# Turning x and the keys of a fused attention and gated kernel on VectorE and through a DRAM scratch instead of on TensorE

## The reference

```python
# r, k, v: (4, 8, 768, 48); w in 0.8..0.95; u: (8, 48)
for t in range(S):
    cur = einsum('bhd,bhe->bhde', u[None] * kt, vt)
    y[:, :, t] = einsum('bhd,bhde->bhe', rt, state + cur)
    state = wt[:, :, :, None] * state + einsum('bhd,bhe->bhde', kt, vt)
x = y.transpose(0, 2, 1, 3).reshape(3072, 384)
xn = x / sqrt(mean(x * x) + 1e-6) * rms_g
x = (silu(xn @ w_gate) * (xn @ w_val)) @ w_out      # 384 -> 1536 -> 384
out = (s * max(x @ w_in, 0) ** 2 + b) @ w_out2      # 384 -> 2048 -> 384
```

## Time and profile before

| | |
|---|---|
| median of 3 runs | 1022.48 us (1021.54 to 1025.43) |
| profiled execution | 1021.45 us |
| its span, first to last instruction | 1019.3 us |
| PE busy | 996.5 us, 98% |
| DVE busy | 523.2 us, 51% |
| ACT busy | 331.4 us, 33% |
| POOL busy | 266.2 us, 26% |
| DMA | 66.12 MB, mean 65 GB/s |
| granted TensorE clock | 1.00 |

### The profile page before, as it was taken

The page is one execution under the profiler, slowest core; times in us unless marked ns, Lnnn a source line. Parts: engine busy times, 40 slices in busy tenths (PEclk is TensorE's granted clock), DMA queues, the critical chain, the costliest instruction groups (busy, mean ns, idle before and its releaser), DMA issues.

```text
span 1019.3 us, 24567 instructions
## 1 busy us (share of the span) xinstructions
PE 996.5 (98%) x10614; PEld 863.9 (85%) x10614; DVE 523.2 (51%) x702; ACT 331.4 (33%) x565; POOL 266.2 (26%) x189
## 2 busy tenths in 40 slices
PE   5899999999999999999999999999999999999998
PEld 5778888888888888888888888898998989989898
DVE  6889836763776477547742225506327054161340
ACT  1442332233223312231323445505226043151340
POOL 4555723551454156316710550000000000000000
PEclk9999999999999999999999999999999999999999
DMA  7570240114013301420104311001010010100000
GB/s 265 163 285 10 83 161 32 49 46 158 33 48 96 138 5 48 147 88 3 49 3 176 103 32 63 0 24 39 17 46 0 23 39 8 54 0 15 15 8 23
DMA packets 21978, 66.12 MB, mean 65 GB/s; under 512 B 2944, under 2 KB 6272, under 8 KB 20608
## 3 DMA queue, kind: packets, MB, share of 16 engines
q1 hardware_dynamic: 21312, 63.65, 17.8%
q10 hardware_dynamic: 576, 1.13, 0.3%
HBM read 55.34 MB, written 9.44 MB: 64 GB/s over the span
## 4 chain that ended last, share of the span: by engine, by line
PE 87%; DVE 1%; issue 0%; ACT 0%; DVEq 0%
PE o_ps L1319 15%; PE o_ps L570 14%; PE value_ps L558 13%; PE gate_ps L558 13%; PE level_ps L47 10%; PE mix_ps L1319 5%; PE gate_ps L47 5%; PE value_ps L47 5%; PE level_ps L430 4%; PE level_ps L504 2%; PE mix_ps L504 2%; PE level_ps L482 1%; PE level_ps L548 0%; PE level_ps L446 0%; PE level_ps L466 0%; PE mix_ps L466 0%
## 5 line engine op out<-in xcount | busy, mean ns | idle before, releaser
L1393 DVE SCALAR_TENSOR_TENSOR sqr<-relu,sb_col 128x512 f32<-128x512 f32 x96 | 72.3, 753 | 216.9 <-ACT relu L1351 216.9
L1108 POOL TENSOR_TENSOR R<-R,arena 128x512 f32<-128x512 f32 x72 | 115.6, 1622 | 196.6 <-PE level_ps L430 175.8
L979 DVE TENSOR_TENSOR u_raw<-value_ps,u_raw 128x512 f32<-128x512 f32 x66 | 45.5, 690 | 126.2 <-PE value_ps L558 126.2
L751 ACT ACTIVATE u_raw<-gate_ps 128x512 f32<-128x512 f32 x72 | 43.0, 598 | 183.4 <-PE gate_ps L558 183.4
L1319 PE MATMUL o_ps<-wt_hi,g_lo 128*128 128x384 f32 x288 | 96.2, 334 | 0.0
L1319 PE MATMUL o_ps<-wt_hi,g_hi 128*128 128x384 f32 x288 | 96.2, 334 | 0.0
L1319 PE MATMUL o_ps<-wt_lo,g_hi 128*128 128x384 f32 x288 | 96.2, 334 | 0.0
L758 ACT ACTIVATE u_hi<-u_raw 128x512 fp32r<-128x512 f32 x66 | 41.7, 632 | 145.6 <-DVE u_raw L979 145.6
L570 PE MATMUL o_ps<-u_hi,wo_hi 128*128 128x512 f32 x216 | 88.4, 409 | 0.0
L558 PE MATMUL value_ps<-x_hi,w_hi 128*128 128x512 f32 x216 | 85.5, 396 | 0.0
L558 PE MATMUL gate_ps<-x_hi,w_hi 128*128 128x512 f32 x216 | 84.7, 392 | 0.7 <-DVE x_lo L952 0.7
(11 more groups left out here) (166 smaller groups left out, 2132.0 us busy)
## 6 DMA issues: line engine op xcount, KB each, us to landing
kr_nat<-kr SPq DMA_DIRECT2D x10, 1152.0 KB, 6.5
K<-kT SPq DMA_DIRECT2D x12, 512.0 KB, 3.9
arena<-wT SPq DMA_DIRECT2D x12, 512.0 KB, 6.7
R<-rT SPq DMA_DIRECT2D x10, 512.0 KB, 4.0
w_raw<-wgv SPq DMA_DIRECT2D x12, 384.0 KB, 6.2
v_sb<-v SPq DMA_DIRECT2D x12, 384.0 KB, 5.2
x_scratch<-x_sb SPq DMA_DIRECT2D x18, 256.0 KB, 2.3
x_raw<-x_scratch SPq DMA_DIRECT2D x6, 768.0 KB, 4.3
```

What stands on the lines that cost most here:

```text
L751: act.activation(u[:, f % 2], gate_ps[:], ACT.Silu).then_inc(silu_done, 1)
L979: dve.tensor_tensor(u[:, f % 2], value_ps[:], u[:, f % 2], ALU.mult).then_inc(u_done, 1)
L1108: pool.tensor_tensor(q, q, decay(blk, l, 0), ALU.mult).then_inc(rmul_done, 1)
L1393: dve.scalar_tensor_tensor(out=sq[f % 2][:], in0=relu[f % 2][:], scalar=sb_col[:, 0:1], in1=relu[f % 2][:], op0=ALU.mult, op1=ALU.mult).th ...
```

## The change

In the stages 1 to 5 neither keys nor x are turned on PE. `turn_keys(s, blk)` on DVE turns 128x1024 keys in blocks of 32 by 32 behind the last key multiplication of each pair (group 18); SP stores the result to `k_scratch` and loads it back in four DMAs of 32 partitions each, which swaps the blocks, 1 KB a piece. KTr is laid out with the pair of heads innermost, so that an update's stationary operand takes every eighth element (`turned_keys`). x goes the same way: `turn(s, blk)`, two DVE operations of 128x384, three stores to `y_scratch` and four loads a pair, in pieces of 256 bytes. The tokens of x then lie in another order (quadrants, blocks inside), which the store of the gated layer's output undoes; the gain g is multiplied in by `upper_x` and `lower_x`. Updates go from behind group 22 to 23, the rest of them and the readings from 24 and 26 to 25 and 27, and what hangs on them. Stage 0 keeps its transposes on PE. Some late weights are split one group earlier.

```diff
-LATE_WEIGHTS = (5, 7, 9, 11, 14, 17, 20, 23, 28)
-LATE_OUT = (8, 13, 16, 21, 27)
+UPDATE_AT, ATTEND_AT, UPPER_AT, NEXT_AT = 23, 25, 33, 34
+LATE_WEIGHTS = (5, 7, 9, 11, 14, 17, 20, 22, 28)
+LATE_OUT = (8, 13, 16, 21, 26)
...
-    KTr = [arena[:, n // C, n % C * NP * P:(n % C + 1) * NP * P] for n in range(CH)]
+    KTr = [arena[:, blk, 0:Q * P] for blk in range(2)]
...
+    def turned_keys(n):
+
+        return KTr[n // C].rearrange("p (d q) -> p d q", q=Q)[:, :, n % C * NP:(n % C + 1) * NP]
+
+    def turned_quadrants(blk):
+
+        return x_raw[:].rearrange("p k (q b f) -> p k q b f", q=QUAD, b=2)[:, :, :, blk]
...
+        def store_turned_keys(s, blk):
+            wait(sp, k_turned, 2 * (s - 1) + blk + 1)
+            wait(sp, kt_in[blk], QUAD * (s - 1) * 16)
+            sp.dma_start(k_dram[blk], KTr[blk].rearrange("p (b f) -> p b f", b=QUAD)).then_inc(kt_stored[blk], 16)
+
+        def load_turned_keys(s, blk):
+            wait(sp, kt_stored[blk], s * 16)
+            for b in range(QUAD):
+                sp.dma_start(KTr[blk][32 * b:32 * b + 32].rearrange("p (a f) -> p a f", a=QUAD),
+                             k_dram[blk, :, b].rearrange("(a i) f -> i a f", a=QUAD)).then_inc(kt_in[blk], 16)
+
+        def store_turned(s, blk):
+            wait(sp, y_turned, CH * (s - 1) + C * blk + C)
+            wait(sp, x_in[blk], QUAD * (s - 1) * 16)
+            for k in range(KT):
+                sp.dma_start(y_dram[blk, k], turned_quadrants(blk)[:, k]).then_inc(y_stored[blk], 16)
+
+        def load_turned(s, blk):
+            wait(sp, y_stored[blk], KT * s * 16)
+            for q in range(QUAD):
+                sp.dma_start(turned_quadrants(blk)[32 * q:32 * q + 32].rearrange("p k q f -> p (k q) f"),
+                             y_dram[blk, :, :, q].rearrange("k (a i) f -> i (k a) f", a=QUAD)).then_inc(x_in[blk], 16)
...
             load_natural(2 * s + 1)
+            for blk in range(2):
+                store_turned_keys(s, blk)
+                load_turned_keys(s, blk)
             if s + 1 < NSB:
                 for blk in range(2):
                     load_keys(s + 1, blk)
...
+            store_turned(s, 0)
+            load_turned(s, 0)
+            store_turned(s, 1)
+            if s + 1 < NSB:
                 load_queries(s + 1, 1)
+            load_turned(s, 1)
+            if s + 1 < NSB:
                 load_values(s + 1, 1)
                 load_natural(2 * s + 2)
...
-            wait(pe, kt_out, turned(CH * s + n) + 1)
-            if n % 2 == 0 and not batch_end(CH * s + n + 1):
-                wait(pe, kt_out, turned(CH * s + n + 1) + (1 if n == 0 else 0))
+            if s == 0:
+                wait(pe, kt_out, 3 if n == 0 else n // 2 * 2 + 2)
+            else:
+                wait(pe, kt_in[blk], QUAD * s * 16)
...
-                                   KTr[n][:, p * P + h * SUB:p * P + (h + 1) * SUB], v_sb[blk][:, c, head * D:(head + 1) * D],
+                                   turned_keys(n)[:, h * SUB:(h + 1) * SUB, p], v_sb[blk][:, c, head * D:(head + 1) * D],
...
         def upper_x(s):
             wait(act, value_done, F1 * s)
+            for blk in range(2):
+                wait(act, x_in[blk], QUAD * s * 16)
             for k in range(KT):
-                wait(act, xe_done, KT * (s - 1) + k + 1)
-                act.activation(x_hi[:, k], x_raw[:, k], ACT.Copy).then_inc(xhi_done, 1)
+                act.activation(x_hi[:, k], x_raw[:, k], ACT.Copy, scale=g_col[:, k:k + 1]).then_inc(xhi_done, 1)
...
+        def turn_keys(s, blk):
+            wait(dve, kmul_done, level_no(s, LV - 1, blk))
+            wait(dve, rmul_done, level_no(s, 1, blk))
+            wait(dve, wb_done, level_no(s, 1, blk))
+            dve.transpose(KTr[blk].rearrange("p (b j q) -> p b q j", b=QUAD, j=32),
+                          K[blk][:].rearrange("p (q b t) -> p b q t", b=QUAD, t=32)).then_inc(k_turned, 1)
+
+        def turn(s, blk):
+            wait(dve, norm_done, CH * s + C * blk + C)
+            wait(dve, xlo_done, split_tiles(s - 1, KT - 1))
+            for c in range(C):
+                out = turned_quadrants(blk).rearrange("p k q (c j) -> p (k q) c j", c=C)[:, :, c]
+                dve.transpose(out, y_sb[C * blk + c][:].rearrange("p (b j) -> p b j", j=32)).then_inc(y_turned, 1)
...
             if k == TOP_AT:
-                keys_after(s, LV - 1)
+                for blk in range(2):
+                    multiply_keys(s, LV - 1, blk)
+                    turn_keys(s, blk)
...
-            if k == 26:
+            if k == ATTEND_AT + 2:
                 normalise(s, 0)
                 attention_out(s, 2)
                 attention_out(s, 3)
-            if k == 28:
+                turn(s, 0)
+            if k == ATTEND_AT + 4:
                 normalise(s, 1)
+                turn(s, 1)
```

More of the change, by code:

```diff
@@ L120, in copied, with by_quadrant, of_block, attention_and_gated_phase @@
     return 2 * (blk + 1) if s == 0 else 2 * (s + 2)
+def by_quadrant(ap, n):
+    return ap.rearrange("p (a n j) -> p a n j", a=QUAD, j=32)[:, :, n]
+def of_block(ap, blk):
+    return ap.rearrange("p (a b f) -> p a b f", a=QUAD, b=2)[:, :, blk]
 def split_tiles(s, k):
     return KT * (s + 1) + k + 1
-def attention_and_gated_phase(nc, block, a, whole, first, x1_dram, x1_out, x_hi, x_lo, const_in_squared, level_ps, mix_ps, gate_ps,
+def attention_and_gated_phase(nc, block, a, whole, first, x1_dram, y_dram, k_dram, x1_out, x_hi, x_lo, const_in_squared, level_ps, mix_ps, gate_ps,
                               value_ps, o01_ps, o_ps):
@@ L221, in attended_ps, with turned_ps @@
         return (first_y_ps if s == 0 else y_ps)[n]
[L223 to L224 removed]
+    def turned_ps(k, blk):
+        return o_ps[k] if blk == 0 else tail_ps[k]
     def natural(b):
@@ L315, in load_keys @@
         def load_keys(s, blk):
-            wait(sp, kt_done, turned(CH * (s - 1) + C * blk + C) if s > 0 else 0)
+            if s == 1:
+                sp.wait_ge(kt_done, C * blk + C)
+            else:
+                wait(sp, k_turned, 2 * (s - 2) + blk + 1)
             sp.dma_start(K[blk][:], a["kT"][2 * s + blk]).then_inc(k_in[blk], 16)
@@ L449, in top_level, with turn_first_keys @@
             mm.then_inc(level_done, 1)
-        def turn_keys(s, n):
-            if batch_end(CH * s + n):
-                return
+        def turn_first_keys(n):
             blk, c = n // C, n % C
[L455 to L458, removed]
+            keys_ready(pe, 0, LV, blk)
+            if n == 3:
                 wait(pe, far_done, copied(0, 0))
[L460 to L463, removed]
             for p in range(NP):
                 q = c * NP + p
-                mm = pe.transpose(keys_ps(s, n)[:, p * P:(p + 1) * P], K[blk][:, q * P:(q + 1) * P], eye[:])
+                mm = pe.transpose(first_kt_ps[n][:, p * P:(p + 1) * P], K[blk][:, q * P:(q + 1) * P], eye[:])
             mm.then_inc(kt_done, 1)
@@ L492, in attend @@
             if blk == 0:
-                wait(pe, kt_out, turned(CH * (s + 1)))
+                wait(pe, kt_out, CH)
+                wait(pe, yo_done, CH * s)
             elif s > 0:
@@ L639, in first_attention @@
             keep_busy(4, gate_ps)
-            turn_x(0, range(0, C))
-            turn_x(0, range(C, CH))
+            first_turn(range(0, C))
+            first_turn(range(C, CH))
             keep_busy(3, gate_ps)
@@ L691, in place_far, with first_keys_out @@
                         act.activation(dst, src[:, :, blk], ACT.Copy).then_inc(far_done, 1)
[L693 to L698, removed]
+        def first_keys_out(n):
+            wait(act, kt_done, n + 1)
+            act.activation(turned_keys(n).rearrange("p d q -> p q d"),
+                           first_kt_ps[n].rearrange("p (q d) -> p q d", q=NP), ACT.Copy).then_inc(kt_out, 1)
         def square(s, n):
@@ L949, in first_lower_x @@
             for k in range(KT):
-                cols = slice(blk * TB, (blk + 1) * TB)
                 wait(dve, xhi_done, KT * blk + k + 1)
-                dve.scalar_tensor_tensor(out=x_lo[:, k, cols], in0=turned_ps(0, k, blk)[:, cols], scalar=g_col[:, k:k + 1],
-                                         in1=x_hi[:, k, cols].bitcast(F32), op0=ALU.mult,
-                                         op1=ALU.subtract).then_inc(xlo_done, 1)
+                dve.scalar_tensor_tensor(out=of_block(x_lo[:, k], blk), in0=of_block(turned_ps(k, blk), blk),
+                                         scalar=g_col[:, k:k + 1], in1=of_block(x_hi[:, k], blk).bitcast(F32),
+                                         op0=ALU.mult, op1=ALU.subtract).then_inc(xlo_done, 1)
         def lower_x(s):
@@ L958, in lower_x, with lower_squared_x @@
                 wait(dve, xhi_done, split_tiles(s, k))
-                dve.tensor_tensor(x_lo[:, k], x_raw[:, k], x_hi[:, k].bitcast(F32), ALU.subtract).then_inc(xlo_done, 1)
+                dve.scalar_tensor_tensor(out=x_lo[:, k], in0=x_raw[:, k], scalar=g_col[:, k:k + 1],
```

(11 more changed lines are left out.)

95 lines of the change are left out of this document (38 added, 57 removed).

## The result

The changed kernel takes 1034.14 us (median of 4 runs, 1033.75 to 1034.53) against 1023.9 (1021.54 to 1025.43, also of 4) for the kernel before on the same chip: ratio 1.0112, 95% interval 1.0096 to 1.0128. It is slower, by 1.1%. The forecast was 1020.5, so its sign is wrong; the stated range, 1010.5 to 1037, holds the time, but only because it was stretched to the rivals; the forecast's own range ended at 1026. The profiled execution took 1033.75 us, its span 1031.6.

A forecast was written before the change was run, and what follows sets the result against it. PE, busy 98% of the span, was taken as the bound; 1021.45 - 13.8 + 7.7 + 2.9 + 2.0 = 1020.3 profiled, given as 1020.5 us. Range 1010.5 to 1037; the forecast's own range 1015 to 1026.

The forecast's parts named there:

- Part 1: Key and x transposes leaving PE behind stage 0: 124 at 0.11 us each, 13.8 us saved.
- Part 2: Updates' weight loads from strided KTr: 24 ns more for each of 320 records, 7.7 us added.
- upper bound of 56 ns a record: Highest price allowed for the updates' strided weight loads, twice the nearest row, 18 us in all.
- Loads hidden: Rival on the updates: strided weight loads cost nothing and stalls are small, 1013 us; chance 0.18.
- Part 3: DVE's key transposes at group 18: 1.2 us each, stages 2 to 5 wait nothing, stage 1 2.9 us once.
- DVE late: Rival at u_lo for group 22: key transpose takes 2.4 us, from strided writes or POOL; 1031 us; chance 0.17.
- Part 4: Keys' way through the scratch: hidden, with 0.7 us to spare for keys 0 and 1.8 for keys 1.
- Part 5: x's way through the scratch to gate 0: slack 0.2 us, 0.4 us of waits per stage, 2.0 in all.
- x late: Rival at gate 0: x_hi waits for the second load; +15 us, 1035, if small pieces halve the rate; chance 0.22.
- both slacks (0.4 and 0.2 us): Spare time forecast for u_lo at group 22 (0.4) and for x's chain through the scratch to gate 0 (0.2).

The follow-up runs named there:

- packed_by_32: The changed kernel with KTr in runs of 32 columns, so an update takes a contiguous stationary operand in 4 matmuls of 32 columns; 1029.16 us, ratio 1.0065.
- packed_by_32_stores_first: The changed kernel with KTr in runs of 32 columns and both stores of x ahead of its loads on SP; 1018.16 us, ratio 0.9959.
- stores_first: The changed kernel with both stores of x ahead of both loads on SP, the next stage's query load behind them; 1027.26 us, ratio 1.0044.
- u_lo_early: The changed kernel with the u_lo of group 22 made between the two key transposes on DVE; 1034.64 us, ratio 1.0117.

## Why the prediction was wrong

- **Part 1** was right: 12.7 us by PE's records where 13.8 was taken.
- **Part 2** had the mechanism and too small a size: 7.7 us at 24 ns a record; the record costs 29 more, 9.3 us. The load grew by 79 ns, not 28: the row used has 12 bytes between elements, 0.44 ns a column, and at 16 and at 32 bytes it is 1.23. The step grew by less than the load. Its price is contained in the upper bound of 56 ns a record. The rival "Loads hidden" is out.
- **Part 3 failed, in the price of the key transposes.** They were taken at 1.2 us, the row of a reduction; they took 2.16, near the upper bound, 2.2. PE wanted u_lo at +6.65 from the first key multiplication (220.98 - 1.06 - 213.27) where +6.5 was forecast, and u_lo ended at +7.7 instead of +6.1. Two other terms of that sum were off too and nearly cancel, which is luck: the multiplications took 2.9 us instead of 2.15, u_lo 0.68 instead of 1.53. For stage 1 the forecast had 2.9 us of waits at three places; 2.3 came, all at the first. For stages 2 to 5 it had none, and 4.2 came. The rival "DVE late" named the place and a cause, writing every eighth element, which packed_by_32 shows to be the one: without the stride the transpose takes 1.25 us beside the same POOL work. The rival gave 2.0 us in each of the stages 2 to 5; 1.0 was measured. 1.2 was a fair price for the operation, for another layout. The reason given for taking the low bound, one operand read, looked at the input; the output has the stride. The Trainium skill's page (VectorE: DVE Perf Modes, The three transpose paths) gave an estimate of 2.5 us, scaled from bf16; the measured 2.16 lies below it, and the 1.25 of a packed output at half of it.
- **Part 4** was right: no wait of PE for keys in the changed kernel. A store lands in 3.1 us, with 3.2 taken. In stage 2 the last load of keys 0 landed at 223.4 for an update at 225.3, that of keys 1 at 228.8 for one at 231.7; less the 1.06 us by which PE was late, that leaves 0.8 and 1.8 us, as forecast. Where PE is less late, this slack shows: packed_by_32 has 0.7 us of such waits.
- **Part 5 failed as well, in the sum of a chain whose slack of 0.2 us was known.** From the first sum of block 1 (244.46) the steps were, forecast and measured: load 0 issued +5.4 and +5.75; its issues over +7.2 and +7.6; load 1 ready +10.4 and +11.4; the first gate matmul +16.2 and +18.0. The time that PE left for it was nearly as forecast (16.4, measured 16.6). The issues of y's stores took 0.63 to 0.67 us each where 0.44 was taken, and the last load landed 3.5 us behind its issue where 2.9 was taken. 6.8 us of waits, against 2.0: the rival "x late" at less than half of its 15. The transfers themselves were no slower than taken: packets of 256 bytes took 19 ns each in the mean in the trace of after (143 ns those of 3 KB, before), so 96 of them are 1.8 us a batch, as forecast (about 2), far from the 13 us of a price by pieces; its 0.8 us for a price by bytes should read 1.1. Whether the longer issues come from the small pieces was not tested (loads of 1 KB pieces went out every 0.43 us), but with the same pieces and both stores first the wait is 0.4 us.
- **The sum** with measured terms: 1021.45 - 12.7 + 9.3 + 6.5 + 6.8 + 2.4 (first matmuls behind waits, clock-keeping matmuls less readings) = 1033.75. Two rivals with 0.17 and 0.22 came true together, each at half its size or less. They had been priced as if only one could; both rested on an optimistic end of a bounded cost, and both slacks (0.4 and 0.2 us) were smaller than the uncertainty of one duration in their chains.

## What to carry to other kernels

When work leaves the engine that bounds a kernel, price what comes back to it: here the keys' part lost by one output layout, which made the loads of the updates longer on PE and the transposes longer on DVE; laid out in runs of 32 it cost hardly anything on either. A slack that is less than the spread of the bounds in its chain is no slack; give such a chain the dearer end in the forecast. In a queue that is served in order, put all that is ready ahead of what must wait for a round trip. An operation that is moved may take another time in its new place, as u_lo did, and a longer wait can cost more than itself where the clock falls behind it; look at both before a reordering is called useless.

## What the hardware showed

- A weight load of 64 fp32 columns takes 138 ns packed and 217 at strides of both 16 and 32 bytes. The step of back-to-back updates went from 30 to 61 ns a record at 32 bytes.
- Matmuls with 32 stationary columns have a load of 110 ns. Twice as many of them took 12.7 us in all in packed_by_32, with waits among them, and 11.7 in packed_by_32_stores_first, where the packed ones of 64 took 11.5.
- DVE's 32 by 32 transposes of fp32: 1.25 us for 128x1024 with a contiguous output, 2.16 with elements written 32 bytes apart, and 0.55 for 128x384 written in runs of 32.
- ACT pays for such a stride in writing too. Its copies of 128x512 out of PSUM, after and before:
```profile
L730 ACT ACTIVATE arena<-mix_ps x1: 1104/1104/1104, 39.4 to 39.4; 128x512 f32<-128x512 f32 x1
```
```profile
L698 ACT ACTIVATE arena<-mix_ps x9: 582/592/597, 39.2 to 505.3; 128x512 f32<-128x512 f32 x9
```
- PE waits for that copy in stage 0 (0.7 us), and behind it the granted clock was lower for a while (stretch, PE busy, clock, DMA share, GB/s; after, then before):
```profile
45.00:50.00 5.00, 5.00 (x69) 0.66 0.05 21
```
```profile
45.00:50.00 5.00, 4.28 (x140) 1.00 0.07 26
```
0.66 over these 5 us is the lower of the two levels, 1.2 GHz, for 3.4 of them. The eight clock-keeping matmuls at 47.70 took 2.07 us instead of 1.16. Other kernels with the same stage 0 (stores_first, u_lo_early) had 1.00 in this stretch, so it is no fixed part of the change's cost. A second such fall, 0.67 from 60 to 65, is in stores_first too (0.66) and not in the kernel before.
